# Moving GpSimd's split of v and its remainder of x to other steps of a hand-ordered attention kernel (Trainium2, one core)

## The reference, cut to what matters

```
q_assign = argmax(q_n . c_n); k_assign = argmax(k_n . c_n)      # 16 clusters a head
scores   = (q k^T) / sqrt(64), set to -1e9 where the clusters differ
attn     = softmax(scores);  out = attn v                        # 2 x 8 heads, 768 tokens, 64 wide
x        = out as (1536, 512)
h        = (x w1) * (x w2);  y = h w3 w_out                      # first block
g        = max(y w_in, 0) + alpha * min(y w_in, 0);  result = g w_out2
```

## Time and profile before

| | us |
|---|---|
| runs | 790.97, 792.37, 791.84 |
| median | 791.84 |
| the profiled execution's own time | 791.99 |
| its span (first to last instruction) | 790.2 |
| TensorE busy in the span | 761.5 |
| VectorE / ScalarE / GpSimd busy | 428.7 / 336.3 / 189.4 |
| longest wait of TensorE on GpSimd in the attention | v (L469): 4.0 in 6 waits |

### The profile page before, as it was taken

One profiled execution on the slowest core, in us unless ns is written; L12 is line 12 of the kernel. 1 busy time (PEld: TensorE's weight loads), 2 busy tenths in 40 slices (PEclk: granted clock), 3 DMA queues, 4 the chain that ended last, 5 costly groups with the idle time before them and its releaser, 6 DMA issues.

```text
span 790.2 us, 12079 instructions
## 1 busy us (share of the span) xinstructions
PE 761.5 (96%) x4290; PEld 712.8 (90%) x4290; DVE 428.7 (54%) x704; ACT 336.3 (43%) x679; POOL 189.4 (24%) x210
## 2 busy tenths in 40 slices
PE   5999999999999998899999999999999999999998
PEld 4887998898899987899999999999999999999997
DVE  5224988889889887542212115467344434443442
ACT  5124988888889787532112114242111112112111
POOL 2120576867767875300000000000000000000000
PEclk9999999999999999999999999999999999999999
DMA  8833464565555322330000003231010001001001
GB/s 284 163 100 98 101 155 105 127 142 127 121 126 134 92 66 63 85 108 1 1 1 0 0 0 107 80 121 67 0 41 1 1 1 40 0 0 40 1 1 40
DMA packets 63577, 54.13 MB, mean 69 GB/s; under 512 B 31264, under 2 KB 51760, under 8 KB 63536
## 3 DMA queue, kind: packets, MB, share of 16 engines
q1 hardware_dynamic: 63536, 53.59, 26.3%
HBM read 31.50 MB, written 3.19 MB: 44 GB/s over the span
## 4 chain that ended last, share of the span: by engine, by line
PE 75%; POOL 15%; issue 5%; DVE 2%; ACT 2%; DMA 1%; POOLq 0%; SPq 0%; ACTq 0%; DVEq 0%
PE slot L575 57%; PE acc L575 14%; POOL xf L520 3%; PE slot L638 3%; POOL xf L516 2%; POOL xl L526 2%; POOL v L469 1%; POOL oh L495 1%; POOL v L465 1%; POOL c L487 1%; POOL c L488 1%; PE slot L689 1%; POOL c L493 1%; POOL c L485 1%; DMA qk<-in_k 1%
## 5 line engine op out<-in xcount | busy, mean ns | idle before, releaser
L575 PE MATMUL slot<-xh,w 128*128 128x384 f32 (+1 forms) x1024 | 277.0, 336 | 0.0
L575 PEld LDWEIGHTS slot<-xh,w 128*128 128x128 f32 x1024 | 186.8, 188 | 2.4
L575 PE MATMUL slot<-xl,w 128*128 (+1 forms) x512 | 172.3, 336 | 0.0
L1027 ACT CAST gh<-gf 128x384 fp32r<-128x384 f32 x64 | 32.9, 514 | 204.2 <-PE acc L575 178.2
L1127 DVE TENSOR_REDUCE nm<-slot 128x1 f32<-128x768 f32 x96 | 91.2, 950 | 22.7 <-PE slot L575 22.3
L1133 DVE TENSOR_TENSOR pl<-slot,ph 128x384 fp32r<-128x384 f32 x192 | 97.6, 550 | 10.6 <-ACT ph L900 10.4
L900 ACT CAST ph<-slot 128x384 fp32r<-128x384 f32 x192 | 83.6, 487 | 35.9 <-PE slot L638 35.4
L575 PEld LDWEIGHTS slot<-xl,w 128*128 128x128 f32 x512 | 96.0, 187 | 2.2
L892 ACT ACTIVATE pf<-slot,nm 128x768 f32<-128x768 f32 x96 | 87.9, 916 | 8.8 <-DVE nm L1127 8.7
L575 PE MATMUL slot<-k,q 96*128 96x384 f32 (+1 forms) x384 | 83.6, 339 | 1.7 <-DVE xl L1089 1.7
L638 PE MATMUL slot<-ident,pf 128*128 128x128 f32 x576 | 81.5, 275 | 2.0 <-DVE pl L1133 1.6
(11 more groups left out here) (121 smaller groups left out, 1113.0 us busy)
## 6 DMA issues: line engine op xcount, KB each, us to landing
stage<-in_moe_w SPq DMA_DIRECT2D x16, 256.0 KB, 3.1
stage<-in_moe_w_in SPq DMA_DIRECT2D x16, 256.0 KB, 2.7
stage<-in_moe_w_out SPq DMA_DIRECT2D x16, 256.0 KB, 3.0
qk<-in_q SPq DMA_DIRECT2D x16, 192.0 KB, 3.9
qk<-in_k SPq DMA_DIRECT2D x16, 192.0 KB, 4.2
vn<-in_v SPq DMA_DIRECT2D x16, 192.0 KB, 3.7
stage<-in_moe_w SPq DMA_DIRECT2D x6, 512.0 KB, 5.3
q<-k SPq DMA_DIRECT2D x16, 192.0 KB, 3.3
```

The lines of the kernel that those rows point to most:

```text
L575: return nc.tensor.matmul(o, a, b, start=start, stop=stop)
L1027: copy(gh[j % 2][:, :], gf[j % 2][:, :]).then_inc(gh_done, 1)
```

## The change

It touches only GpSimd's stream. `split_v` moves from c % 6 = 2 of the head itself (c = 6 j + 2) to the last step of the head in front of it (c = 6 j - 1); head 0's split stands ahead of the first step. The remainders of the first heads of a pair (heads 0 and 2 of a turn) move from c = 16 and 28 to c = 21 and 33, behind the scaling of the second head (c = 20 and 32); the remainders of heads 1 and 3 stay in c = 22 and 34. ScalarE, VectorE, TensorE and SyncE are unchanged, the wait of L905 with them.

```diff
+def remainder_now(c):
+
+    j, u = divmod(c - T6 - LX, T6)
+    return j - 1 if j in (1, 3) and u == 3 else j if j in (1, 3) and u == 4 else None
...
                     normalise(it, out_head, 0)
                 if u == 2:
                     normalise(it, out_head, 1)
-                if t == 2 and (not last or j < HB):
-                    split_v(it, j)
+                if t == 5 and (not last or j + 1 < HB):
+                    split_v(it, j + 1)
                 if c == LEAD and not last:
                     pool.wait_ge(prep_full, FILLS * (2 * it + 2))
                     for h in range(HB, 2 * HB):
                         window(it, h)
-                if split_now(c) is not None:
-                    x_lo(it, split_now(c))
+                if remainder_now(c) is not None:
+                    x_lo(it, remainder_now(c))
...
             picks(0, 0, 1)
             picks(0, 0, 2)
+            split_v(0, 0)
             for c in range(LEAD):
                 step(0, c, False)
```

## The result

The changed kernel takes 859.57 us (median of 4 runs, 858.39 to 862.27), against 792.11 us of the kernel before on the same chip: a ratio of 1.0841, 95% interval [1.0806, 1.0877]. It is 67 us slower. The forecast was 857.3 with a range from 845 to 869. The profiled execution took 858.39 us, with a span of 856.6 against 790.2.

A forecast was written before the change was run, and what follows sets the result against it. TensorE was taken to bound the attention. From the profiled 791.99: -1.0 early split, +36.2, +17.2 and +2.5 stops, +1.0 start, +9.6 clock gave 857.5, or 857.3 against the median; range 845 to 869.

The forecast's parts named there:

- What bounds the kernel: Attention: TensorE bounds it, matmuls filling 29.7 of a pair's 30.9 us; GpSimd is just in time, not full.
- Part 2, the stops: Steps 20 and 32: ScalarE's copy waits for the moved remainder, seven stops; +36.2 us looped, +17.2 turn 2, +2.5 turn 3.
- Part 1, the early split: First weigh of a head: v split earlier gains 0.2 us in each of six places, -1.0 us.
- Part 3, the start: Start: head 1's split between first and second picks delays VectorE's step 8, +1.0 us once.
- Part 4, the clock: Behind each of six long stops TensorE runs at half clock, 1.6 us each, +9.6 us.
- Turn 3: Last turn, no picks left: one short stop of 2.5 us, with no clock loss behind it.
- the first block: Remainders of heads 14 and 15 end about 1 us later, long before the second token block reads them: no cost.
- The clock that holds: Rival: the stops come but TensorE's clock holds behind them, 847.7 us; chance 0.15.
- the clock that stays low twice as long: Rival: clock low twice as long behind stops, or a later wait pushed too, 867 us; chance 0.13.
- faster: Rival: the wait of L905 is not met late; 787.8 us if the copy also came earlier; chance 0.03.
- no change: Rival: both moves are hidden, 792 us; chance 0.03.

The follow-up runs named there:

- the kernel with sums in xo: The whole change, with each head's sum and scaling written to xo so ScalarE's copy waits for no remainder, against the kernel before: 792.35 us.
- the late x_hi alone: Kernel before, with ScalarE's x_hi of heads 0 to 2 one step later, behind the output copy: 790.8 us.
- two of the three: Change with sums in xo and x_hi one step later: 790.35 us; kernel before with x_hi and VectorE's reciprocal one step later: 790.96 us.
- with all: The change with sums in xo, x_hi of heads 0 to 2 one step later and VectorE's reciprocal one step later: 786.49 us.
- the kernel with the 40 matmuls: The change, with 40 unread matmuls put in TensorE's stream ahead of the weigh of steps 20 and 32: 853.95 us.
- the kernel with the splits alone: Kernel before, with the splits of v moved as in the change and the remainders left in place: 806.37 us.

## Why the prediction was right

**What bounds the kernel** held in part. GpSimd is in the chain by being just in time, but that is a bound too: TensorE is busy 29.7 of a pair's 30.9 us, and where gaps were taken away without GpSimd's new order the looped pair stayed at 30.8 to 30.9 us, with the wait for v grown from 0.57 to 1.5. The gaps in the earlier trace rows are 1.2 us a pair, not "about 1.5".

**Part 2, the stops,** is confirmed in mechanism, number and size. Seven waits on the remainder, 54.0 us; taken away by other data placement, the loss is gone (792.35); with the split ahead of it, it grows by 1.45 to 2.0 us a time (870.92); moved back in every other pair, only those pairs are free of it (837.48). The size: 9.05 and 8.6 us forecast, 8.84 and 8.50 measured. GpSimd's instructions ran a little faster in the stop: the remainder took 1.80 instead of 1.84 us, the scaling 2.19 instead of 2.25. The step that decided the forecast was to compare, within one step number, the time at which GpSimd ends (185.19) with that at which ScalarE begins (178.32): program order alone shows the remainder only one step late.

**Part 1, the early split:** "The gain is 0.2 us in each of the six places" shows in the kernel with sums in xo (0.9 us over the six), but not in the change, where the gaps are 0.62 to 0.95 us with ScalarE's x_hi and copy last to come, 0.4 us more than before over the six. That term, -1.0 us, was wrong for the change itself. What the text did not see at all is that this split, placed there without part 2, would cost 14 us. It counted each part against the kernel before, and was spared the error because the change makes both.

**Part 3, the start:** +1.0 forecast, +1.0 measured, and the gap is in all kernels with the moved split and the reciprocal in its old place (0.65 to 0.68 us idle in step 10, the rest behind it).

**Part 4, the clock:** the row at the end of the attention priced it near enough. In place of one 3.4 us stretch at 0.50, there are 10.2 us a stop, of which 4.3 to 5.4 fall behind it. That loses 2.0 to 2.5 us at first, more than the 1.6 reckoned, and 0.3 to 0.8 come back as TensorE's small waits in the next steps are covered, which the forecast did not have. Net of that, 9.3 us for the six against 8.6 forecast (9.6 and -1.0): the mechanism is right, that the size is so near is partly luck. That the clock is a term of its own is shown by the pairs of 39.2, 40.7 and 41 us.

The Trainium skill, page "TensorE: Matmul & The Clock Gate", section "HAM oscillation — how this bites in real kernels", describes a kernel whose bursts of matmuls are parted by waits and each begin at the half clock. Behind each of the six long stops this trace agrees; the estimate by its price, 10.2 us, was as good as mine.

**Turn 3** was mis-sized: "nothing for the short one". The stop was 2.5 us as reckoned, but the clock fell behind it too (3.4 us at 0.50), and again for 6.8 us behind two gaps of 1.6 and 0.95 us, which the kernel before has as well, at 1.00. This cost 4.1 us. At the end of the attention 2.4 us came back: the idle time there was 1.5 instead of 2.4 us and no stretch at 0.50 followed it. The 1.2 us of the first block, forecast as nothing, are told in the last section. The terms left out (+4.1, -2.4, +1.2, and -1.6 by the start of the execution) and the 1.0 us short of the long stops nearly cancel; that the whole is within 2.3 us of the median is luck to that extent.

**The rivals.** The clock that holds (847.7) and the clock that stays low twice as long (867) lie on both sides of what happened; faster and no change did not come about.

## What to carry to other kernels

Before an instruction is moved back in one engine's stream, list every wait that its semaphore ends on the other engines, and compare clock times, not step numbers: an engine that lags by 6 us in the same step turns a move of one step into a stop of 9 us. A buffer's release is such a wait, and it is dangerous where it stands first in an in-order step that feeds the bottleneck; the same release waited for on a queue with slack cost nothing that could be measured (792.35 against 792.41). And what is late behind a lagging engine is a row of consumers: moving the first one away only hands the bill to the next, so gains appear when the lag itself and the consumers are treated together (792 with the sums in xo alone, 791 with the late x_hi alone, 790 and 791 with two of the three, 786.5 with all). Whether a gap of the bottleneck is worth closing shows in the length of the repeated stretch, not in the gap.

## What the runs showed of the hardware that was not expected

**GpSimd and VectorE wait for each other.** In the change the remainders of heads 14 and 15 come back to back at the end of the attention and overlap two of VectorE's remainders of w. The timeline of the change, and then of the kernel with head 2's remainder back in step 28, where one of GpSimd's is already done:

```profile
399.18 4.83 POOL L532 TENSOR_TENSOR xl<-xf,xh 64x768 fp32r<-64x768 f32 x2
...
401.07 4.01 DVE L1199 TENSOR_TENSOR w<-stage,w 128x1024 fp32r<-128x1024 f32 x2 [6.72 <-ACT w L966]
```

```profile
379.06 1.85 POOL L532 TENSOR_TENSOR xl<-xf,xh 64x768 fp32r<-64x768 f32 x1 [1.01 <-ACT xh L918]
...
380.02 3.11 DVE L1199 TENSOR_TENSOR w<-stage,w 128x1024 fp32r<-128x1024 f32 x2 [5.97 <-ACT w L966]
```

The second remainder took 2.9 us instead of 1.84, VectorE's pair 4.01 instead of 3.11, and the 0.9 us reach TensorE: the +1.2 us in the table, which the second kernel does not have. Its 3.11 us are not undisturbed either: the first of the pair took 1.98 of them beside the remainder. How long the same work of VectorE takes alone, and beside GpSimd's scaling, shows in two more places of the change:

```profile
377.77 2.21 POOL L526 TENSOR_TENSOR xf<-xf,rep 64x768 f32<-64x768 f32 x1
...
378.12 2.94 DVE L1199 TENSOR_TENSOR w<-stage,w 128x1024 fp32r<-128x1024 f32 x1 [0.39 <-ACT w L966]
...
407.68 1.23 DVE L1199 TENSOR_TENSOR w<-stage,w 128x1024 fp32r<-128x1024 f32 x1 [0.39 <-ACT w L966]
```

It takes 1.23 us alone. Beside the scaling it ends at 381.06, 1.08 us after GpSimd's end at 379.98, and GpSimd's own 2.21 us are not longer than elsewhere. In seven such overlaps, three here and four in the kernel before, the one that started second ended about its own length after the end of the first: they took turns. The Trainium skill, page "GPSIMD Engine Reference", section "8. Key points", says that GpSimd shares its SBUF interfaces with VectorE and contends with VectorE instructions that have two SBUF inputs, as this one has; the rows agree, with a wait for the whole of the other instruction.

**The clock fell behind short pauses too.** In the kernel with the 40 matmuls it went to 0.50 for 3.4 us behind three of the four stops that left TensorE 1.9 us idle, and behind neither of the two that left 1.7. In the kernel with the splits alone it fell behind one of the four gaps of 2.0 us.

**The start differs between executions.** The same matmuls at 24 us were between 1.6 us early and 2.0 us late of the kernel before. The 1.6 us of the change are one stretch of the clock, here in the kernel before and then in the change:

```profile
16.30:19.70 3.40, 3.40 (x9) 2.66 (x10) 3.40 (x4) 2.29 (x3) 0.00 (x0) 0.50 1.03 367
```

```profile
16.30:19.70 3.40, 3.40 (x16) 2.77 (x17) 3.40 (x4) 2.10 (x2) 0.00 (x0) 1.00 1.03 345
```

A difference of one or two microseconds between two profiled executions of this kernel is therefore no evidence by itself.
